# Sixth and seventh slot of a fused attention, token mixing and gating kernel: order of x's copies on ScalarE, low parts of token pieces exchanged between VectorE and GpSimd, channel mixing waiting for u by thirds

## The reference

```python
# 1. attention with a decayed state, per head
state = alpha[t][:, None] * state + outer(k[t], v[t]);  y[t] = q[t] @ state
# 2. token mixing and channel mixing
theta = x @ w_theta
y = w_tok_r @ (x * cos(theta)) + w_tok_i @ (x * sin(theta))     # over the tokens
u = x + y
x = u + maximum(u @ w_ch, 0)
# 3. gated feed forward with a spatial product
h = maximum(x @ w_in, 0);  u, v = halves(h)
out = (u * (w_spatial @ normalise(v) + b_spatial[:, None])) @ w_out
```

## Time and profile before

| what | value |
|---|---|
| median of 3 runs | 580.37 us (580.26 to 580.7) |
| the profiled execution: its own time | 581.29 us |
| the profiled execution: its span | 579.5 us |
| TensorE busy in the span | 566.0 us (98%), 5806 matmuls |
| VectorE busy | 396.9 us (68%) |
| ScalarE busy | 246.7 us (43%) |
| GpSimd busy | 226.5 us (39%) |
| granted clock of TensorE | 0.999 of full speed |

### The profile page before, as it was taken

How to read it: one execution, slowest core, us unless ns; L and a number is a source line. 1 busy time by engine, 2 the same in 40 slices (tenths; PEclk the granted TensorE clock), 3 DMA queues, 4 the chain that set the end, 5 groups by cost and what they waited for, 6 DMA issues and landing times.

```text
span 579.5 us, 13709 instructions
## 1 busy us (share of the span) xinstructions
PE 566.0 (98%) x5806; PEld 538.6 (93%) x5806; DVE 396.9 (68%) x626; ACT 246.7 (43%) x461; POOL 226.5 (39%) x184
## 2 busy tenths in 40 slices
PE   6899899999999999999999999999999999999997
PEld 5787799999999999999999989999999899989997
DVE  6988999788776766876544379978437852776253
ACT  2767555453544544545442226822432243134210
POOL 2356442442332522523422047463813481347131
PEclk9999999999999999999999999999999999999999
DMA  7952222232322332323033180200220022002002
GB/s 285 338 197 93 90 94 73 80 102 70 110 70 70 115 112 91 112 70 110 3 114 119 42 286 1 81 1 1 82 83 1 0 83 81 1 2 82 1 1 81
DMA packets 21229, 49.69 MB, mean 86 GB/s; under 512 B 1712, under 2 KB 16816, under 8 KB 20656
## 3 DMA queue, kind: packets, MB, share of 16 engines
q1 hardware_dynamic: 21168, 48.81, 24.2%
HBM read 39.37 MB, written 9.44 MB: 84 GB/s over the span
## 4 chain that ended last, share of the span: by engine, by line
PE 84%; DVE 9%; ACT 2%; POOL 2%; issue 1%; DMA 1%; DVEq 0%; ACTq 0%
PE psY L535 19%; PE psC L567 6%; PE psC L491 5%; PE psY L712 4%; PE psY L663 4%; PE psS L431 3%; PE psY L673 3%; PE psF L653 3%; PE psS L712 3%; PE psF L712 3%; PE psY L653 2%; PE psS L663 2%; PE psS L673 2%; PE psF L673 2%; PE psF L466 2%; PE psC L712 2%
## 5 line engine op out<-in xcount | busy, mean ns | idle before, releaser
L1381 POOL TENSOR_TENSOR z_lo<-cos_sin,z_hi 128x768 fp32r<-128x768 f32 x23 | 43.8, 1906 | 87.0 <-ACT z_hi L830 87.0
L1455 POOL TENSOR_TENSOR gated_lo<-raw_gated,gated_hi 128x384 fp32r<-128x384 f32 x32 | 35.9, 1126 | 70.4 <-ACT gated_hi L979 69.2
L1368 POOL TENSOR_TENSOR akq<-akq 128x512 f32<-128x512 f32 x23 | 27.3, 1188 | 70.7 <-DVE akq L1046 70.7
L1388 POOL TENSOR_TENSOR u_lo<-u_f,u_hi 128x384 fp32r<-128x384 f32 x24 | 29.2, 1245 | 46.1 <-ACT u_hi L835 46.1
L979 ACT ACTIVATE gated_hi<-raw_gated 128x384 fp32r<-128x384 f32 x32 | 16.4, 527 | 58.0 <-DVE raw_gated L1290 57.4
L535 PE MATMUL psY<-tok_r_hi,z_hi 128*128 128x384 f32 x117 | 41.0, 350 | 0.0
L1449 POOL TENSOR_TENSOR vn_lo<-raw_vn,vn_hi 128x512 fp32r<-128x512 f32 x24 | 33.7, 1423 | 17.0 <-ACT vn_hi L957 17.0
L535 PE MATMUL psY<-tok_i_hi,z_lo 128*128 128x384 f32 x117 | 39.2, 335 | 0.0
L535 PE MATMUL psY<-tok_i_lo,z_hi 128*128 128x384 f32 x117 | 39.2, 335 | 0.0
L535 PE MATMUL psY<-tok_r_hi,z_lo 128*128 128x384 f32 x117 | 39.2, 335 | 0.0
L535 PE MATMUL psY<-tok_i_hi,z_hi 128*128 128x384 f32 x117 | 39.1, 335 | 0.0
(11 more groups left out here) (309 smaller groups left out, 1839.6 us busy)
## 6 DMA issues: line engine op xcount, KB each, us to landing
akq<-akq SPq DMA_DIRECT2D x22, 770.0 KB, 4.5
v<-v_in SPq DMA_DIRECT2D x24, 192.0 KB, 4.6
x_dram<-u_f SPq DMA_DIRECT2D x8, 576.0 KB, 3.6
out<-ot SPq DMA_DIRECT2D x24, 192.0 KB, 1.9
raw_x<-x_dram SPq DMA_DIRECT2D x3, 1152.0 KB, 5.0
raw_tok_r<-w_tok_rT SPq DMA_DIRECT2D x6, 384.0 KB, 7.3
raw_tok_i<-w_tok_iT SPq DMA_DIRECT2D x6, 384.0 KB, 8.3
raw_sp<-w_spT SPq DMA_DIRECT2D x4, 576.0 KB, 6.2
```

The source lines that it names most:

```text
L1381: pool.tensor_tensor(Z[c][1][:], trigs[g % 2][:], f(Z[c][0][:]), ALU.subtract).then_inc(z_lo, 1)
L1455: pool.tensor_tensor(GA[1][:, j, half(h)], ug[:, j, half(h)], f(GA[0][:, j, half(h)]), ALU.subtract).then_inc(g_lo, 1)
```

## The change

Pieces 5 and 7 change engines for their low part: 5 goes to VectorE, 7 to GpSimd. TensorE's waits for pieces now name both pieces of a pair (`wait_tok`). On ScalarE, in slot 5, `copy_x`, `xT_high` and `sines` stand ahead of the high parts of pieces 6 and 7, and `whole_turns(5)` and `copy_kT(6)` come from slot 6 into slot 5, ahead of `keep_xT(5)`. In slot 6 `copy_x(6)` stands ahead of `z_high(5)`. On VectorE, in slot 6, `xT_low(6)` stands ahead of `scale_keys(7)` and `decay_queries(7)`. On GpSimd the piece after `z_low(3)` is gone, and piece 7 comes after `z_low(4)`. In channel mixing the first of three tiles waits for the three parts of `u_lo` one by one, before the three matmuls that read each; the second and third tile don't wait for it.

```diff
-MID_SPLITS = (6, 7, 8, 9)
+MID_SPLITS = (5, 6, 8, 9)
+LOW_SPLITS = (0, 1, 2, 3, 4, 7, 10, 11)
...
+            def wait_tok(i):
+                if i in MID_SPLITS:
+                    pe.wait_ge(tok_lo_mid, MID_SPLITS.index(i) + 1)
+                else:
+                    pe.wait_ge(tok_lo, LOW_SPLITS.index(i) + 1)
+
             def first_mix(unit, tiles, parts):
...
                 if parts == Z_HIGH:
-                    pe.wait_ge(tok_lo, s // 2 * 2 + 2)
+                    wait_tok(s // 2 * 2)
+                    wait_tok(s // 2 * 2 + 1)
...
             def channel_mix(n, angles_before, bank=psC):
...
-                pe.wait_ge(u_lo, (n // CT + 1) * CT)
                 if bank is psC:
                     need(pe, x2_made, n)
                 need(pe, angled, angles_before)
                 for j in range(CT):
+                    if m_out == 0:
+                        pe.wait_ge(u_lo, n // CT * CT + j + 1)
...
@@ ScalarE, first loop
                 if c == 1:
                     tok_high(SPLITS[0][1])
-                if c == CHUNKS - 1:
-                    for i in SPLITS[c]:
-                        tok_high(i)
                 copy_x(c)
...
                     sines(c - 1)
                 if 1 < c < CHUNKS - 1:
                     xT_high(c)
+                if c == CHUNKS - 1:
+                    for i in SPLITS[c]:
+                        tok_high(i)
                 if c > 1:
                     z_high(c - 1)
+                if c == CHUNKS - 1:
+                    whole_turns(c)
+                    copy_kT(c + 1)
                 if c:
                     keep_xT(c)
...
@@ ScalarE, second loop
-                    if g < AHEAD:
+                    if g == CHUNKS:
+                        sines(g - 1)
+                        copy_x(g)
+                        z_high(g - 1)
+                    elif g < AHEAD:
                         whole_turns(g - 1)
...
@@ VectorE, second loop
-                    if g < AHEAD:
+                    if g == CHUNKS:
+                        reduce_angle(g - 1)
+                        mask_scores(g)
+                        multiply_z(g - 1)
+                        decays_back(g + 1)
+                        xT_low(g)
+                        scale_keys(g + 1)
+                        decay_queries(g + 1)
+                    elif g < AHEAD:
                         reduce_angle(g - 1)
...
                         make_x2(tile_of(b, c))
-                        xT_low(g)
+                        if g > CHUNKS:
+                            xT_low(g)
...
@@ GpSimd
             z_low(CHUNKS - 3)
-            tok_low(CHUNKS - 1)
             scale_queries(CHUNKS)
             z_low(CHUNKS - 2)
+            tok_low(CHUNKS + 1)
```

More of the change, by code:

```diff
@@ L522, in token_mix @@
                 if k < HALVES:
[L523 to L527, removed]
+                    wait_tok(k * CHUNKS + s // 2 * 2)
+                    wait_tok(k * CHUNKS + s // 2 * 2 + 1)
                 if h == 0:
```

## The result

The first comparison gave a ratio of 0.9932 (95% interval 0.9919 to 0.9945): 580.37 x 0.9932 = 576.4 us, under the forecast of 577.7 and just under the range, which began at 576.8. Its median was 577.16 us beside 580.54 for the kernel before. The kernel is 3.3 to 3.9 us faster; 2.7 was forecast.

What follows compares the result with a forecast made beforehand. TensorE's waits in slots 5 and 6 were taken to bound the kernel. 2.68 us there, less 0.3 in slot 7, plus 0.3 for u, make 2.7: from 580.37 to 577.7 us, range 576.8 to 579.3.

Steps and rivals of the forecast that it cites:

- Slots 5 and 6: TensorE's stalls in these two slots shrink, so that it leaves slot 6 earlier by 2.68 us.
- the late copy of `x`: Slot 5, ScalarE: copying x ahead of the token pieces removes the transposes' whole stall, 0.78 us.
- the held `scale_keys(6)`: Slot 5, VectorE: without GpSimd's piece 5 it takes 0.69 instead of 1.85 us; 0.38 us of the angles' stall stays.
- the stall at the attention: Slot 6: TensorE's wait for the masked scores, 0.87 us with overlap; 0.37 is gained and 0.50 stays.
- `z_high(5)` behind `copy_x(6)`: Slot 6, ScalarE: the z copy goes after x; cost taken as 0, with 0 to 1.0 us kept for the range.
- second and fourth rival: Slot 6: GpSimd's piece 7 holds multiply_z(5), 578.7, 20%; z_low(4) and piece 7 get ahead of VectorE's pieces, 582.0, 5%.
- the place of `xT_low(6)`: Slot 6, VectorE: ahead of scale_keys(7) and decay_queries(7), it removes the angles' stall, 0.56 us.
- ScalarE's orders: Slots 5 and 6: earlier x copies and earlier turns on ScalarE, worth 0.78 + 0.37 + 0.59 us.
- `x` ahead of z in slot 6: Slot 6, ScalarE: x copied at attention's end removes all of the transposes' stall, 0.59 us.
- Slot 7 gives some back: Slot 7: VectorE comes only 2.30 us earlier where 2.5 is needed, so the angles wait; 0.3 us lost.
- Third rival: Slot 7: VectorE sets its end whatever TensorE does; only 0.18 us of slack and 0.3 for u stay, 579.9, 8%.
- u by thirds: Channel mixing, last u_lo set of the MoE part: waiting part by part removes the 0.2 us stall, 0.3 with overlap and restart.

Runs made afterwards that it cites:

- xT5_late6: The changed kernel with xT_low(5) ahead of decay_queries(6) and piece 6's low part moved behind multiply_z(5) on VectorE; ratio to the kernel before 0.994.
- xT5_first: The changed kernel with xT_low(5) put between scale_keys(6) and decay_queries(6) on VectorE in slot 5; ratio to the kernel before 0.998.

## Why the prediction was right or wrong, point by point

- **Slots 5 and 6 were right, place by place.** Forecast 2.68 us, measured 2.62. In slot 5 the late copy of `x` and the held `scale_keys(6)` had the sizes and the causes given (0.74 and 0.40). Of the stall at the attention, a half stays, as forecast (0.28 shown and 0.17 of overlap; 0.50 forecast). `z_high(5)` behind `copy_x(6)` cost nothing: second and fourth rival did not come. Piece 7 on GpSimd ended at +14.06, 0.08 after `multiply_z(5)` had been issued, and that one took 0.96 us.
- **But a term of the sum is not the value of its edit.** Taken out singly, the exchange costs 1.18 us at slot 7's start, the place of `xT_low(6)` 1.19, both of ScalarE's orders 0.96 (0.56 of it for slot 6). The sum, 3.3, is more than the 2.62 that they bring together. My sum took the edits together and in order, and so it held. Read as the price of one edit, a wait shown in the trace before was right once (0.59 for `x` ahead of z in slot 6, 0.56 measured), too low once (0.56 for `xT_low(6)`) and too high once (1.74 for ScalarE's orders).
- **The first step that failed: "Slot 7 gives some back", 0.3 us; it gave 0.04.** VectorE's lead at `xT_low(7)` (how much earlier it comes than before) was put at 2.30 us; measured it is (88.13 - 53.06) - (84.83 - 52.29) = 2.53, and TensorE, whose own lead there is 35.29 - 32.70 = 2.59, needed only 2.59 - 0.18 = 2.41. 0.18 of the missing 0.23 is one wait that I had read as VectorE's own pace: before, the reduction started 1.44 us behind the start of w_ch's low part since the turns were not there; after, 1.26 (73.62 to 74.88), straight behind it. `multiply_z(6)` took 0.96 as forecast. Third rival: it did not come here, but with less slack `xT5_late6` shows slot 7 to slot 8 lengthening to 13.68.
  The reduction of the kernel before, on VectorE, and the turns from ScalarE that it waited for (77.17 + 0.52 = 77.69, and the next instruction starts at 77.73):

```profile
76.29 1.35 DVE L1178 TENSOR_TENSOR ch_lo<-raw_ch,ch_hi 128x1152 fp32r<-128x1152 f32 x1
77.73 0.56 DVE L1079 SCALAR_TENSOR_TENSOR psC<-turns,psC 128x384 f32<-128x384 f32 x1
```

```profile
77.17 0.52 ACT L810 ACTIVATE turns<-turns 128x384 f32<-128x384 f32 x1
```

- **The second: "u by thirds", 0.3 us; it brought 0.73.** I put the one row of the wait view down to the last set of u parts, in what the prediction calls the MoE part (the first part of the kernel, to about 340 us). It belongs to the set before. The two tiles, before and after:

```profile
311.41 0.44 PE L567 MATMUL psC<-u_hi,ch_hi 128*128 128x384 f32 x1 [0.15 <-POOL u_lo L1388]
...
336.18 0.44 PE L567 MATMUL psC<-u_hi,ch_hi 128*128 128x384 f32 x1
```

```profile
307.78 0.33 PE L573 MATMUL psC<-u_hi,ch_hi 128*128 128x384 f32 x1
...
332.18 0.33 PE L573 MATMUL psC<-u_hi,ch_hi 128*128 128x384 f32 x1
```

  Both first matmuls lasted 0.44 us before and 0.33 after. The second stall, the one for the set of the earlier trace rows, which ends at 336.13, is in no list, for its idle time behind the matmul before (335.72 + 0.39 = 336.11) is only 0.07 us; yet it lost overlap and restart. In the traces' own times, 0.77 us of it from the start, TensorE's lead is 3.30 us ahead of the first tile, 3.77 behind it and 4.11 behind the second. So the stall in the list cost 0.47 us, where my term had 0.3 (0.2 with overlap and restart, 0.17 + 0.11, would by my own count have been 0.48), and a stall outside the list cost 0.34.
- **The range.** The two steps together are 0.26 + 0.43 = 0.7 us more than forecast, and slots 5 and 6 gave 0.06 less. The places of the trace give 2.58 + 0.73 = 3.3 us, so 577.1. That lies inside the range, whose lower end was 0.9 below the forecast, and the five later rounds give the same. What took the first comparison below 576.8 is that it read another 0.6 us lower. That fits the spread of the start, for which the range left no room: the changed kernel's four times were 576.68 to 577.17, while the later rounds have 576.70 to 578.38, and the one of them that is profiled, 577.86, is of the late sort. Which sorts those four runs were is seen in a trace for one of them only, so this share is argued, not shown.

What is not settled: what decides whether TensorE's matmuls of the first slot run in 1.16 or 2.08 us, and whether its clock falls at 25 us. It was not tried, since no part of the change touches it.

## What to carry to other kernels

Count times from the last place that the change doesn't touch, not from the start of the span: here that took a spread of 1.1 us out and left 0.04. A stall of TensorE, whose matmuls overlap, costs more than its idle time shows, and a stall with nearly no idle time is still one: look for first matmuls that last longer than their kind. Before an instruction is made earlier, ask which instruction of the engine that it shares a lock with it will meet then; the order of six such instructions was worth 1.7 us here, more than any single wait of slots 5 and 6.

## What the runs showed of the hardware

- VectorE and GpSimd instructions with their operands in SBUF hold each other: `scale_keys` took 0.68 to 0.69 us where it was not held, 1.15 to 2.23 beside `z_low` or a piece on GpSimd; `z_low` 1.81 to 1.86 where it was not held, 2.47 to 2.80 behind VectorE's pieces or its scan (`decays_back`). Where both engines had instructions waiting they alternated (`xT5_first`). `mask_scores`, with one operand in PSUM, took 1.20 to 1.23 us in every trace, also beside a GpSimd piece (52.92 beside 52.62 in the kernel before).
- The time that an instruction is held is part of its own duration and stands in no list of waits: it shows only beside an instruction of the same kind that was not held.
- The stretch of TensorE matmuls from 8 to 12 us, the first scores and the ten matmuls behind them, took 1.16 + 1.32 or 2.08 + 2.15 us in different executions of one kernel, at a granted clock that the rows show as 1.00 both times, and that sets the whole kernel off by 1.1 us.
- In 2 of 13 executions TensorE's granted clock fell to 0.50 at 25 to 27 us, behind 1.46 us of idle time that all 13 have; a 128x384 matmul then took 0.52 instead of 0.33 us, and slot 4 came 0.3 to 0.6 us later.
